# A fused attention, expert and LayerNorm kernel: value products turned round, row sums on ScalarE, their reciprocals spread by DMA

## The reference, cut to what matters

```python
# q, k, v: [2, 8, 768, 64]; n_global = 8, n_local = 96
scores = q @ k.T / sqrt(64)
bias   = -slope[h] * dist                 # 96 for the 8 global keys outside the window, else |distance|
scores = where(keep, scores + bias, -1e9) # keep: 8 first keys, or the last 96 keys of the query
a      = exp(scores - max);  a = a / (sum(a) + 1e-9)
x      = (a @ v) as [1536 tokens, 512]
# experts, e = 0..3, p = domain_probs / (sum + 1e-9)
out    = sum_e p[:, e] * (relu(x @ w1[e]) @ w2[e])
# last part
h      = out @ w_in;  solu = h * softmax(h);  ln = (solu - mu) / sqrt(var + 1e-6) * g_ln
result = ln @ w_out                       # [1536, 512]
```

## Time and profile before

| what | us |
|---|---|
| median of 3 runs | 737.36 (737.16 to 737.41) |
| the profiled execution | 737.83 |
| its span, first to last instruction | 736.0 |
| TensorE busy | 732.3 (99%) |
| VectorE busy | 513.3 (70%) |
| ScalarE busy | 224.0 (30%) |
| GpSimd busy | 351.6 (48%) |

### The profile page before, as it was taken

One profiled execution on the slowest core, in us unless ns is written; L12 is line 12 of the kernel. 1 busy time (PEld: TensorE's weight loads), 2 busy tenths in 40 slices (PEclk: granted clock), 3 DMA queues, 4 the chain that ended last, 5 costly groups with the idle time before them and its releaser, 6 DMA issues.

```text
span 736.0 us, 12608 instructions
## 1 busy us (share of the span) xinstructions
PE 732.3 (99%) x3992; PEld 651.1 (88%) x3992; DVE 513.3 (70%) x1031; ACT 224.0 (30%) x421; POOL 351.6 (48%) x395
## 2 busy tenths in 40 slices
PE   9999999999999999999999999999999999999998
PEld 8888899889998899998899988999889888888887
DVE  5777768766676765767767677676677658767773
ACT  5677642111111111111111211111124465433322
POOL 4567546436253462524526255261529986442400
PEclk9999999999999999999999999999999999999999
DMA  8735310100110000100001100000033000000001
GB/s 227 238 106 155 107 31 1 58 30 30 28 58 28 28 28 28 57 28 28 28 28 50 35 28 28 28 28 0 0 115 115 0 1 15 15 30 28 18 27 43
DMA packets 38227, 36.12 MB, mean 49 GB/s; under 512 B 14512, under 2 KB 31152, under 8 KB 38192
## 3 DMA queue, kind: packets, MB, share of 16 engines
q1 hardware_dynamic: 36448, 33.46, 14.4%
q10 hardware_dynamic: 1744, 2.23, 0.9%
HBM read 32.54 MB, written 3.15 MB: 48 GB/s over the span
## 4 chain that ended last, share of the span: by engine, by line
PE 98%; DVE 1%; issue 0%; POOL 0%; ACT 0%; DVEq 0%
PE y_ps L895 35%; PE p_ps L875 32%; PE o_ps L942 5%; PE pT_ps L923 3%; PE s_ps L913 3%; PE up_ps L1123 3%; PE up_ps L1121 3%; PE up_ps L1122 3%; PE out_ps L1151 2%; PE out_ps L1153 2%; PE out_ps L1152 2%; PE lnT_ps L1136 1%; PE xt_ps L953 1%; PE xr_ps L1036 1%; PE o_ps L1012 1%; DVE ex L1933 0%
## 5 line engine op out<-in xcount | busy, mean ns | idle before, releaser
L895 PE MATMUL y_ps<-w2s,hs 128*128 128x512 f32 x1140 | 265.4, 390 | 0.0
L895 PEld LDWEIGHTS y_ps<-w2s,hs 128*128 128x128 f32 x1140 | 213.4, 188 | 43.4 <-issue 0.3
L875 PE MATMUL p_ps<-xs,ws 128*128 128x384 f32 x1344 | 240.1, 335 | 0.0
L875 PEld LDWEIGHTS p_ps<-xs,ws 128*128 128x128 f32 x1344 | 234.5, 188 | 2.6
L1614 DVE SCALAR_TENSOR_TENSOR acc<-y_ps,pr,acc 128x512 f32<-128x512 f32 x178 | 132.8, 749 | 65.6 <-PE y_ps L895 61.7
L1233 ACT ACTIVATE hs<-hs_sum 128x384 fp32r<-128x384 f32 x128 | 67.4, 527 | 147.7 <-DVE hs_sum L1579 81.8
L1598 DVE SCALAR_TENSOR_TENSOR hs<-hs_sum,hs 128x384 fp32r<-128x384 f32 x128 | 94.8, 741 | 19.7 <-ACT hs L1233 19.6
L681 POOL CAST w2s<-raw_sum 128x1024 fp32r<-128x1024 f32 x16 | 16.7, 1041 | 172.0 <-PE y_ps L895 172.0
L1228 ACT ACTIVATE kept<-p_ps 128x384 f32<-128x384 f32 x32 | 15.8, 493 | 232.2 <-PE p_ps L875 232.2
L1246 ACT ACTIVATE neg_s<-neg_s,row 128x256 f32<-128x256 f32 (+1 forms) x96 | 42.3, 484 | 27.2 <-DVE row L1636 27.0
L1565 DVE TENSOR_TENSOR hs_sum<-p_ps,kept 128x384 f32<-128x384 f32 x32 | 17.9, 558 | 42.8 <-PE p_ps L875 42.5
(11 more groups left out here) (207 smaller groups left out, 1018.0 us busy)
## 6 DMA issues: line engine op xcount, KB each, us to landing
raw_sum<-in_w SPq DMA_DIRECT2D x28, 512.0 KB, 3.2
qk<-in_qkW SPq DMA_DIRECT2D x16, 256.0 KB, 3.1
qk<-in_qkW SPq DMA_DIRECT2D x31, 128.0 KB, 3.2
v_sb<-in_v SPq DMA_DIRECT2D x16, 192.0 KB, 3.1
out<-o_sb SPq DMA_DIRECT2D x11, 256.0 KB, 2.0
raw_sum<-in_w ACTq DMA_DIRECT2D x4, 512.0 KB, 5.9
raw_sum<-in_w_in SPq DMA_DIRECT2D x1, 2048.0 KB, 7.7
wout_lo_a_sum<-in_w_out SPq DMA_DIRECT2D x1, 1792.0 KB, 7.5
```

Source lines behind the costliest of these rows:

```text
L875: mm = nc.tensor.matmul(bank, ws[slot][:, w, part, kk, :], xs[:, 2 * bt + kk, x, part, :], start=(kk == 0 and w == 1 and x == 1), stop=(kk ...
L895: mm = nc.tensor.matmul(mixed_at(s, t), hs[ring][:, h, b, tok], w2s[slot][:, w, f, :], start=(f == 0 and h == 1 and w == 1), stop=(f == 1 ...
```

## The change

1. **Value products turned round.** v (64 columns, no column of ones) is the weight, the transposed probabilities (128 columns) are moved. The two heads go to column halves of the array and so to partition halves of the output, which comes out as [head and feature, token]: the six transposes of `turn_pair` and `xt_ps` are gone. `o_ps` is now two tiles of two banks, used in turn by the pairs.
2. **Row sums on ScalarE.** Each exponential gives its row sum with `accum_out`. VectorE adds 1e-9 and takes reciprocals (`shares`) in the first step of the next pair, behind its second `add_bias`.
3. **Spread by DMA.** TensorE transposes the [128, 12] reciprocals at the head of the second step (`turn_shares`), VectorE copies the 12 rows, SP writes them to DRAM, waits, and loads them back over 64 partitions for each head in two DMAs (`spread_shares`, in the SP order behind that step's `load_qk` and ahead of `load_v`).
4. **Normalising.** One multiply of [128, 2, 384] for each pair (`normalise`), from PSUM straight into the sums of x; in the first step of the pair after the next, behind `shares`.
5. **Splitting x.** VectorE makes the three sums alone; ScalarE makes hi parts from SBUF, three blocks in one instruction; GpSimd makes all seven lo blocks and starts only when all four sums are there.
6. **Copies of `pT_ps`.** Three by VectorE and three by ScalarE for each pair, two and four before.
7. **The seam.** `turn_shares` between products 1 and 2; expert step 1 now waits for lo block 0 of the last pairs at its product 1 (`xs_lo` 13), and does mixes 0 to 2 ahead of product 2. On VectorE three `add_up` stand ahead of `first_block`.
8. **The end.** The two last tiles are only centred before the transposes and the product; the scale is worked out later and put on in ScalarE's copy of the result.

```diff
-    ACT_COPIES = 4 * PAIRS
-    DVE_COPIES = 2 * PAIRS
+    ACT_COPIES = 3 * PAIRS
+    DVE_COPIES = 3 * PAIRS
...
+                def spread_shares(r):
+
+                    sp.wait_ge(shares_copied, r + 1)
+                    sp.wait_ge(normed, START + r)
+                    sp.dma_start(shares_dram[r], share_rows[:, :]).then_inc(shares_out, 16)
+                    sp.wait_ge(shares_out, 16 * (r + 1))
+                    for m in range(2):
+                        sp.dma_start(shares_sb[m * D:(m + 1) * D, :, :].rearrange("p a c -> p (a c)"),
+                                     shares_dram[r, m * QB:(m + 1) * QB, :].rearrange("i q -> (i q)").partition_broadcast(D)
+                                     ).then_inc(shares_in, 16)
+
+                for n in range(BL * OUTER):
+                    if n + BL < BL * OUTER:
+                        sp.wait_ge(scored, START + STEP_TILES * (n + 1))
+                        load_qk((n + BL) // STEPS_PAIR, n % BL)
+                    if n % STEPS_PAIR == 1 and n > 1:
+                        spread_shares(n // STEPS_PAIR - 1)
...
+                pool.wait_ge(xs_sum, START + 4 * j + 4)
+                for n, blocks in enumerate(((0,), (1, 3), (5, 6, 4), (2,))):
+                    pool.wait_ge(xs_hi, START + 4 * j + n + 1)
...
+                    out = o_ps[p][:, i // 3, i % 3 * P:(i % 3 + 1) * P]
                     for half in range(0 if i else 1, 2):
                         at = i - 1 if half == 0 and i > 1 else W + i + half - 1
-                        mm = nc.tensor.matmul(o_ps[:, m, i * DV:(i + 1) * DV],
-                                              pT[c % 2][:, e, (2 * m + half) * P:(2 * m + half + 1) * P],
-                                              v_sb[:, p, m, at, :], start=(half == 0 or i == 0), stop=(half == 1))
...
+                        for head in range(2):
+                            mm = nc.tensor.matmul(out[head * D:(head + 1) * D, :], v_sb[:, p, head, at, :],
+                                                  pT[c % 2][:, e, (2 * head + half) * P:(2 * head + half + 1) * P],
+                                                  start=(half == 0 or i == 0), stop=(half == 1))
...
+            def turn_shares(j, q):
+
+                pe.wait_ge(row_step, START + 2 * PAIRS * j + 2 * q + 2)
+                pe.wait_ge(normed, START + PAIRS * j + q)
...
             def attention_step(j, b):
+                if b % STEPS_PAIR == 1 and begun(j, b - STEPS_PAIR):
+                    turn_shares(j, b // STEPS_PAIR - 1)
...
-                if b % STEPS_PAIR == STEPS_PAIR - 1 and begun(j, b - STEPS_PAIR):
-                    turn_pair(j, b // STEPS_PAIR - 1)
...
                 product(0, 1, 0, 0, 0, 0)
+                turn_shares(OUTER, -1)
                 product(0, 2, 0, 0, 0, 0)
                 values(OUTER, -1)
-                product(0, 6, 0, 0, 0, 0)
-                product(0, 7, 0, 0, 0, 0)
-                turn_pair(OUTER, -1)
-                for n in (5, 4, 3):
+                for n in (6, 7, 5, 4, 3):
                     product(0, n, 0, 0, 0, 0)
...
+                pe.wait_ge(xs_lo, START + 13)
                 product(s, 1, i, g, slot, bt)
+                for t in range(3):
+                    mix(last, t, last_slot, ring, last_g)
+                pe.wait_ge(xs_lo, START + 14)
                 product(s, 2, i, g, slot, bt)
...
-                nc.scalar.activation(tile, tile, ACT.Exp, bias=row[:, b // STEPS_PAIR, m, i:i + 1], scale=-1.0
-                                     ).then_inc(exp_ready, 1)
+                nc.scalar.activation(tile, tile, ACT.Exp, bias=row[:, b // STEPS_PAIR, m, i:i + 1], scale=-1.0,
+                                     accum_out=sums[:, b // STEPS_PAIR, m, i:i + 1]).then_inc(exp_ready, 1)
...
             def attention_step(j, b):
-                if b % STEPS_PAIR == STEPS_PAIR - 1 and begun(j, b - STEPS_PAIR):
-                    normalise(j, b // STEPS_PAIR - 1)
                 if not (isinstance(j, int) and j == 0 and b < 2):
+                    if b % STEPS_PAIR == 1 and begun(j, b - STEPS_PAIR):
+                        copy_shares(j, b // STEPS_PAIR - 1)
                     for t, i, e, m in tiles(b):
                         add_bias(j, b, t, i, e, m)
+                        if b % STEPS_PAIR == 0 and t % STEP_TILES == 1:
+                            if begun(j, b - STEPS_PAIR):
+                                shares(j, b // STEPS_PAIR - 1)
+                            if begun(j, b - BL):
+                                normalise(j - 1, b // STEPS_PAIR)
...
                 if b == 0 and begun(j, -1):
-                    even_sums(j - 1, halves[0])
+                    even_sum(j - 1)
                 if b == STEPS_PAIR and begun(j, -1):
-                    odd_rest(j - 1, whole)
-                if b == STEPS_PAIR + 1 and begun(j, -1):
-                    odd_sums(j - 1, *halves)
+                    odd_sums(j - 1)
...
+                normalise(OUTER - 1, 0)
+                shares(OUTER, -1)
                 copy_pT(OUTER, -1, 1)
-                even_sums(OUTER - 1, halves[0])
+                copy_shares(OUTER, -1)
+                even_sum(OUTER - 1)
                 first_block(0, 0)
                 relu_lo(0, 0, 0)
-                normalise(OUTER, -1)
                 second_sum(0, 0)
                 third_sum(0, 0)
-                odd_rest(OUTER - 1, whole)
                 last_block(0, 0)
                 fourth_sum(0, 0)
                 relu_lo(0, 3, 0)
+                normalise(OUTER - 1, 1)
+                odd_sums(OUTER - 1)
...
+            def centred(s):
+
+                m = s % 2
+                dve.wait_ge(tail_step, linked[0])
+                nc.vector.tensor_scalar(ex[:, m], ex[:, m], mv[:, m, 0:1], None, ALU.subtract).then_inc(ln_ready, 1)
```

More of the change, by code:

```diff
@@ L134, in attention_experts_solu_kernel @@
         ident = sb(base, "ident", [P, P])
+        with ExitStack() as same:
+            shares_sb = sb(same, "shares_sb", [P, 2, NB])
+            share_rows = sb(same, "share_rows", [2 * QB, P])
         wout_hi_a = sb(base, "wout_hi_a", [P, WOUT_SOON, DM], F32R)
@@ L298, in attention_experts_solu_kernel @@
         pT_ps = [ps(pa, f"pT_ps{i}", [P, 512]) for i in range(2)]
-        o_ps = ps(pa, "o_ps", [P, 2, 512])
-        xt_ps = ps(pa, "xt_ps", [P, 1024])
+        o_ps = [ps(pa, f"o_ps{i}", [P, 2, 512]) for i in range(2)]
         pa.close()
@@ L490, in wait_copied @@
                 return
[L491 to L498, removed]
+            if copied_by_dve(e):
+                eng.wait_ge(copied_dve, START + DVE_COPIES * j + b + 1)
             else:
-                eng.wait_ge(copied_act, START + ACT_COPIES * j + 4 * pair + (e + 1 if k == 0 else k + 2))
+                eng.wait_ge(copied_act, START + ACT_COPIES * j + b + 1)
         block = base.enter_context(nc.Block())
@@ L1272, in _, with even_hi @@
[L1272 to L1281 removed]
+            def even_hi(j):
+                act.wait_ge(normed, START + PAIRS * j + 1)
+                nc.scalar.activation(x_blocks(j)[:, 7, :], x_sums(j)[:, 0, :], ACT.Copy).then_inc(xs_hi, 1)
@@ L1355, in _ @@
                 for j in range(OUTER):
[L1356 to L1360 removed]
+                    even_hi(j)
+                    odd_hi(j)
+                    sums_hi(j)
+                    last_sum_hi(j)
                 halve(0, 0)
@@ L1645, in copy_pT, with shares @@
                 nc.vector.tensor_copy(pT[b % 2][:, e, :], pT_ps[e][:, :]).then_inc(copied_dve, 1)
-            def copy_first_pT():
-                dve.wait_ge(turned, START + 2)
-                nc.vector.tensor_copy(pT[0][:, 1, :], pT_ps[1][:, :]).then_inc(first_copied, 1)
+            def shares(j, q):
+                at = 2 * PAIRS * j + 2 * q
+                dve.wait_ge(exp_ready, START + UL * j + U * q + U)
+                at_least(dve, shares_turned, PAIRS * j + q)
+                nc.vector.tensor_scalar(sums_eps[:, :, :], sums[:, q % 2], 1e-9, None, ALU.add).then_inc(row_step, 1)
+                dve.wait_ge(row_step, START + at + 1)
+                nc.vector.reciprocal(share[:, :, :], sums_eps[:, :, :]).then_inc(row_step, 1)
@@ L1816, in first_halve @@
             def first_halve(s, i, bt, last_bt, expert, first):
+                for t in range(3):
+                    add_up(s - 1, t, last_bt, expert, first)
                 first_block(s, i)
-                add_up(s - 1, 0, last_bt, expert, first)
                 relu_lo(s, 0, bt)
-                add_up(s - 1, 1, last_bt, expert, first)
-                add_up(s - 1, 2, last_bt, expert, first)
                 second_sum(s, i)
```

254 lines of the change are left out of this document (113 added, 141 removed).

## The result

The changed kernel takes 746.48 us (744.62 to 747.15) where the kernel before takes 737.36 (737.16 to 737.41), both medians of 5 runs. The ratio of the runs is 1.0118, 95% interval 1.0106 to 1.0129: slower by 9.1 us, where I had forecast 3.6 us less and a range up to 741. The profiled execution took 745.55 us with a span of 743.7, against 737.83 and 736.0: +7.7 us between the two traces.

The account below looks back on a forecast made before the run. TensorE, busy for 99% of the span, was taken as the bound. Terms -4.9 (three passes), -2.8 (first pass), +3.8 (seam), -0.6 (end), +0.9 (spread) gave -3.6: 737.36 to 733.8 us, range 729 to 741.

Parts of the forecast that it names:

- Rivals 2 and 3: Value products: column halves take turns, 741 us, chance 0.12; their weight loads aren't hidden either, 760 us, chance 0.04.
- floor of 8.95: Attention: TensorE's own time in us for a pair after the change, against 11.2 before; a pass 17.9.
- A steady pass: Attention, six steps (two pairs): 21.1 us against 22.75, -1.65 each, three times -4.9.
- both latenesses: Steady pass: VectorE's copy and sums make the bias 0.8 us late, ScalarE's three block hi part delays exponentials by 0.5.
- The insert: Pair's first step: shares and normalise between second and third add_bias make that step 4.07 us and a pair 9.9.
- Rival 1: Attention: VectorE's inserted step overlaps with waits counted in full; a pass near 19.5 us, 729 in all, chance 0.15.
- The first pass: Start of attention: four steps without normalise at some 3.1 us for 3.8, -2.8.
- The spread: Shares through DRAM: 7.8 us, wanted at 9.0, so hidden by 1.2; first pairs beside expert weights add 0.9 in all.
- Rival 4: Spread is late: loads land in 5.9 us, normalise 1.6 late in each of seven pairs, +11, 745; chance 0.07.
- Rival 5: Seam: TensorE's clock falls after standing 3.6 us, +3, 737, no difference; chance 0.12.
- The seam: Attention's end to product 1 of expert step 1: 16.2 us against 12.4, TensorE stands 3.6, +3.8.
- The end: Last tiles: centring removes TensorE's waits of 0.8 and 0.2 us, -0.6, between 0 and -0.9.

Follow-up runs that it names:

- e7: Changed kernel with VectorE's sums behind a pair's second step, shares and normalise behind the fourth bias, transposed shares in unused PSUM columns: 742.37 us.
- e2: Changed kernel without the DMAs that spread the shares, x multiplied by a constant: 745.08 us.
- e10: Changed kernel with 45 useless transposes between first and second pass and 26 ahead of product 1 of expert step 1: 743.70 us.
- e4: Changed kernel with GpSimd making the lo part of block 0 after the even sum, not behind all four sums: 746.46 us.
- e1: Kernel before with only the end of the change (last two tiles centred, scale applied in ScalarE's output copy): 736.98 us against 737.54.
- e3: Changed kernel with three of the four first expert weight loads issued later, from SP's queue ahead of attention steps 9, 12 and 15: 742.83 us.
- e9: As e8, with last lo parts before a weight split on GpSimd, lower block before normalise on VectorE, mix 3 before product 6 on TensorE: 733.74 us.
- e8: Changed kernel with the changes of e3, e4 and e7, reordered seam work on ScalarE and VectorE, shares' write ahead of q and k loads: 738.53 us.
- e12: As e9, with the three late weight loads back on ScalarE's queue, together behind the first pass: 738.58 us.

## Why the prediction was wrong, by its own steps

1. **Bound and TensorE's price: right.** Column halves run at once and hide their loads; 1.02 and 0.81 us were forecast as 1.03 and 0.81. Rivals 2 and 3 fall. On rival 3 the Trainium skill, TensorE: Matmul & The Clock Gate, Part 3, says that a weight load overlaps with running products only where the row group differs. The trace disagrees: column halves of one row group, 16 records of 128 columns in 1.02 us, changeover included, are at the rate of 8 whole-array transposes (1.02). The floor of 8.95 was not reached: the shortest pairs take 9.55 and 9.58 (e7), and without its waits for ScalarE, 0.75, the latter would be 8.83.
2. **A steady pass: 0.5 short, and nearer than its parts.** 21.6 against 21.1, but the pairs were forecast as 9.9 and 11.2 (with both latenesses in the second) and measured 10.76 and 10.84. The first is 0.9 longer, and its `normalise` waits 0.95 us for a spread that I had as hidden by 1.2: each link was short (write 2.06 against 1.7, loads 4.32 against 3.1, SP's issues). That two errors of opposite sign leave 0.5 is luck. It is `turn_shares`, waiting for `normalise`, that TensorE stands for, not the scores. The insert counts, but how much isn't separated (e7). Rival 1 falls.
3. **The first pass: right on TensorE.** The scores of step 7 begin at 20.80 us, 23.63 before: -2.8. The mark at step 6 shows only -1.5, since the exponentials now end 1.4 us behind that start, where they ended with it before. Counted by these starts, the two steps behind the pass lose 9.1 us (scores of step 9 at 37.2 against 30.9).
4. **The spread: this step failed.** "For the first pairs, while the expert weights come (5.9), I add 0.9 in all" measured +8.1 over two steps, 9 times as much. I had the row of the 512 KB loads and took their time for an upper bound. But 5.9 is their median: in the trace before, the four land 4.3, 5.3, 6.5 and 7.2 us behind their issues, and SP sends nothing between 21.6 and 31.1 us, so that no row had a small load behind them. Here the spread's load, issued behind three of them, takes 8.15, the write ahead of it pays again (4.02 instead of 1.7), and SP could not even issue it while it sent q and k (1.73). The bound should have been the sum over the chain of dependent transfers with each at its worst. Rival 4 had the right mechanism with the wrong weights: it charged 1.6 us to each of seven pairs; the first waits 7.1, and of the others two wait 0.45 and 0.95.
5. **The clock: weighed, at one place only.** Rival 5 gave it 3 us at the seam, and the forecast 1.00 throughout. It fell three times. Where a second engine sets the pace, TensorE stands 1 to 2 us somewhere, and that was followed by half clock at 94 us here and twice in e2, but not each time (see the last section). The Trainium skill, TensorE: Matmul & The Clock Gate, Part 1, prices it as the time at the lower rate times one half; by that, an estimate, the changed kernel would lose 6.8 us for its 13.7. The runs show less: e10 gets back 2.8 us with 10.2 us of it removed. TensorE also stands in part of that time (from 29.0 to 32.4 us, for one).
6. **The seam: right in size, incomplete in cause.** +3.6 against +3.8, a stand of 3.3 against 3.6, released by GpSimd as forecast. But the sum had no half clock and the 3.6 have 3.4 us of it in them, so the match is in part luck, and mix 0's wait lay hidden right behind (e4), because I did not ask what is queued behind `normalise` on VectorE.
7. **VectorE's sums: priced by rows that read PSUM.** 0.55 each by the earlier trace rows; from SBUF they are 0.54 to 1.43. That made the last step's scores 1.67 us late (92.17), and the second fall of the clock came behind it.
8. **The end: right**, -0.6 in both traces and in e1.

Sum by terms, forecast and measured: first pass -2.8, -1.5; spread +0.9, +8.1; three passes -4.9, -1.9 (of which -2.1 in the first two, the third lost by the clock at 94 us); seam +3.8, +3.6; end -0.6, -0.6. In all -3.6 and +7.7. Of the 11.3 us between them the spread is 7.2, the three passes 3.0 (a steady pass 0.5 to 0.6 short, twice, and the late scores and the clock in the third) and the first pass 1.3, by the marks; the seam is 0.2 better. By the starts of the scores the 1.3 belong to the spread too. Not settled is how the clock's loss divides over the stretches of one run, since it differs from run to run, nor how a steady pass divides between the insert and the spread.

## What to carry to other kernels

A kernel that is gapless on TensorE gives up more than the stand when another engine takes over the pace: a stand of one to a few us can be followed by a stretch at half clock. So when a change takes time off TensorE, see first which waits come up, and move work off the engine that becomes the bound in the same change.

A transfer that something waits for must be priced where it is slowest, by the slowest row and not the median, with every dependent DMA of its chain and the queue that issues it; bulk loads without a near due time belong behind it. And when a wait is taken away, look at the next instruction's wait of the same length before costing the gain.

## What the runs showed of the hardware

- A dependent write of 6 KB took 4.02 us (4.55 in e3) beside one load of 512 KB, and the spread's load of 192 KB behind it 8.15, behind three more, at a DMA share of 0.85 (0 to 20 us) and 0.69 (20 to 40). The load took 4.31 with those three away and 3.3 (median of the issues) at the seam; in steady pairs write and load took 2.06 and 4.32 (57 to 64 us).
- VectorE's subtraction of 128x384 with both inputs in SBUF takes 0.55 us while GpSimd waits (109 us) and 0.96 to 1.43 beside GpSimd's casts and copies (the lines at 88 to 91 us); at 46 us it takes 0.55 and GpSimd's bias of 128x384 beside it 1.07, the next one 0.58; with one input in PSUM it was 0.552 to 0.554 at any time before. The Trainium skill, SBUF — State Buffer, section "SBUF: two separate sides", says that a VectorE operation with two SBUF inputs and a GpSimd operation exclude each other; the trace agrees with these durations, and by that sentence the term could have been given a higher bound ahead of the run.
- The length of a stand alone doesn't tell whether half clock follows. Stands of 1.66 us (e3, 88 us), 1.73 (e2, 84 us) and 1.76 (e9, 97 us) were not followed by it; one of 1.67 (changed kernel, 90 us) was, and one of 1.05 (e8, 58 us; half clock from 61.0). In e12 the time varies by 9.9 us and the mean clock from 0.995 to 0.986, which is worth some 6.7 us at most (an estimate: half of the time at half clock, from mean clocks and spans), so something else varies too; the gapless kernel before stays within 1.4.
- With 71 transposes that nothing reads (e10) the kernel took 743.70 us instead of 746.48.
